# Last dense block of a fused attention and mixture-of-experts kernel: gate logits of its last five hidden tiles through a folded weight product, and their down matmuls in the first routing search

## The chip, the cores and the metric

One core of one Trainium2 chip. The metric is the device time of the whole kernel in microseconds (us); lower is better. TensorE (PE in the profile) does matrix products, VectorE (DVE) and ScalarE (ACT) elementwise work, GpSimd (POOL) indirect transfers and small tables, SyncE (SP) issues most DMAs.

## The reference, cut to what matters

```python
# x: 3072 tokens x 384, out of a linear-attention recurrence
h = np.maximum(x @ w_in, 0.0)             # dense block, w_in 384 x 2048
x2 = h * h @ w_out                        # w_out 2048 x 384
logits = x2 @ w_gate                      # 384 x 8
order = np.argsort(-logits.flatten())     # greedy assignment, every expert takes 384 tokens
for idx in order:
    tok, e = idx // E, idx % E
    if assigned[tok] >= 0 or counts[e] >= cap: continue
    assigned[tok] = e; counts[e] += 1
out[mask_e] = np.maximum(x2[mask_e] @ w1[e], 0.0) @ w2[e]     # w1 384 x 1024, w2 1024 x 384
```

The routing has to follow exactly computed logits, so every float32 operand of the big products is split into a high and a low part, and each product is three matmuls (high·high, high·low, low·high).

## The kernel before, in words

There are three stages. In the opening and the "blocks" the attention of chunk c runs beside the dense block of chunk c-1. Chunks have 128 positions of 4 sequences, so a dense block has 512 token columns; there are six (m = 0 to 5). A dense block is 16 hidden tiles of 128: `up(m, q, s)` is 9 matmuls into PSUM bank `U[s % 2]`, ScalarE takes the Relu (`hr`, line 725), VectorE squares it (line 953), ScalarE writes the high part `HH` (line 709) and VectorE the low part `HL` (line 965), both in rings of `HRING` = 4 tiles. `down(m, s)` is 9 matmuls into the three accumulators `ACC[0..2]`, `LAG` = 2 steps behind `up` (line 1448). Beside that, each step of the blocks c = 2 to 6 splits half a piece of an expert's weights into high and low (lines 709 and 973) and SyncE stores it to DRAM. `TERMS` lists the three parts of a product.

In the last call of `body` (c = 6, the dense block of chunk 5; `att` is false) steps 0 and 1 do `up(5, ., 0)` and `up(5, ., 1)` with the last two downs of the block before, and steps 2 to 15 do `up(s)` and `down(s - 2)`. The last two downs stand behind the body as a loop of its own (line 1476). At the steps 3, 5, 7 and 9 the rows of the block before are transposed (line 1417), and at step 3 its logits are computed (12 float32 matmuls with the 32 padded columns of `wg`, line 1379).

Then `ACC` goes to `x2T` by ScalarE and VectorE, `logits(0..2)` makes 12 float32 matmuls into `LAST_T`, VectorE copies them to `LT`, TensorE transposes them (line 1627), and VectorE takes them into `Lm` (line 1206). From there the first routing search runs (`r` = 0): for each of six levels of bits VectorE compares all keys with thresholds (line 1033), TensorE counts with 24 small bfloat16 matmuls (`count`, line 1506), VectorE finds which counts are full (line 1044), TensorE sums that (`digit_of`, line 1514), VectorE takes the digit and goes down a level. After the last level come `tie` (lines 1518, 1520), `owned` (1524), `slots` (1531) and the row indices `rowidx` (line 1141). Between these small steps TensorE is given matmuls without a use (`keep_warm`, line 1288; `warm_up`, line 1283) and the transposes of the last block's x2 rows, one of four for each level (`transpose_x2`, line 1483). ScalarE copies each and stores it with a DMA of its own queue to `x2_dram` (line 806, semaphores `st_last`).

GpSimd waits for `st_last` and for `rowidx`, then gathers expert 0's 384 rows in three indirect DMAs (line 676). TensorE transposes each (line 1541), they are split, and the expert's tiles begin (line 1572 for the first, 1595 and 1608 for the rest), with the later searches between them. SyncE waits for `st_last` (line 576), then for `widx` (which expert it is, line 1071), and loads that expert's pieces 0 and 1 of both parts; it then waits for all three gathers before pieces 3, 4 and 2. Expert 0's pieces go to the first 6144 columns of `WH` and `WL`, where the dense up weights were.

Of the kernel before, what the change touches and what calls it, by code (L numbers as in the profile page):

```python
# [53 lines left out]
MOST = NT - 6  # L54
TAB_STEPS = 18
# [9 lines left out]
def bass_attention_moe_routed_moe(nc, rk_in, tok_in, wT_in, urow_in, dw_in, w_gate, ew_in,  # L65
                                  tri_in, pcol_in, rows_in, masks_in, x2_dram, wh_dram, wl_dram, out):
# [19 lines left out]
    with ctx:  # L86
# [105 lines left out]
        x2last = [rk_flat[:, (CB + n) * DM:(CB + n + 1) * DM] for n in range(2)]  # L192
# [71 lines left out]
        acc_mm = sem("acc_mm")  # L264
        logit_mm = sem("logit_mm")

# [110 lines left out]

        def chunk_at(s, att, moe, post):
# [93 lines left out]
        LAST_T, LAST = U[0][:, 0:BATCH * EP], U[0][:, BATCH * EP:2 * BATCH * EP]  # L472
# [6 lines left out]
        def _(sp):  # L479
# [119 lines left out]
        def _(pool):  # L599
# [45 lines left out]
            pool.wait_ge(st_done, NT)  # L645
            pool.iota(iota, [[1, 128]], base=1, channel_multiplier=0,
# [60 lines left out]
        def _(act):  # L707
# [8 lines left out]
            def body(c, q, att, moe, post):  # L716
                m = c - 1
                for s in range(NF1):
                    if moe and post and s == LAG:
                        evacuate(m - 1)  # L720
                    if moe:
# [5 lines left out]
                        after(act, down_mm, g - HRING + 1)  # L727
                        copy(HH[:, s % HRING, :], hr[:, s % 2, :]).then_inc(hh_done, 1)
                    for n, kind, b in tasks_at(s, att, moe, post):
                        task(c, q, P[n % 3], kind, b)  # L730
# [66 lines left out]
            act.wait_ge(acc_mm, 1)  # L797
            copy(x2T[:, 0, :], ACC[0][:, :]).then_inc(acc_act, 1)
            act.wait_ge(acc_mm, 3)
            copy(x2T[:, 2, :], ACC[2][:, :]).then_inc(acc_act, 1)  # L800
            for b in range(BATCH):
                act.wait_ge(x2_mm, EARLY + b + 1)
                after(act, st_last[b % 2], 16 * (b // 2))
                copy(x2last[b % 2], x2_bank(b)).then_inc(row_done, 1)
                act.wait_ge(row_done, EARLY + b + 1)
                act.dma_start(x2_dram[b * SEQ + (NC - 1) * CHUNK:b * SEQ + NC * CHUNK, :],
                              x2last[b % 2]).then_inc(st_last[b % 2], 16)
# [45 lines left out]
        def _(dve):  # L853
# [91 lines left out]
            def body(c, q, att, moe, post):  # L945
                m = c - 1
                for s in range(NF1):
                    if moe and post and s == LAG:
                        evacuate(m - 1)
                    g = NF1 * m + s  # L950
# [5 lines left out]
                    for n, kind, b in tasks_at(s, att, moe, post):  # L956
                        task(c, q, P[n % 3], kind, b)
# [5 lines left out]
                    if moe:  # L963
                        dve.wait_ge(hh_done, g + 1)
                        tt(HL[:, s % HRING, :], hr[:, s % 2, :], HH[:, s % HRING, :].bitcast(f32),  # L965
                           ALU.subtract).then_inc(hl_done, 1)
                    if chunk_at(s, att, moe, post) is not None:
# [6 lines left out]
                    if moe and not att and s == 11:  # L974
                        dve.wait_ge(rt_go, 16 + NLEV)
                        nc.vector.tensor_copy(upperb, upper[:, :]).then_inc(tab, 1)
                        dve.wait_ge(lg_done, NC - 1)
# [221 lines left out]
            dve.wait_ge(x2_mm, EARLY)  # L1199
            dve.wait_ge(acc_mm, 2)  # L1200
            nc.vector.tensor_copy(x2T[:, 1, :], ACC[1][:, :]).then_inc(acc_dve, 1)
            dve.wait_ge(tab, TAB_STEPS + 1)
            dve.wait_ge(logit_mm, 1)
            nc.vector.tensor_copy(LT[:, :], LAST_T).then_inc(lt_done, 1)
# [71 lines left out]
        def _(pe):  # L1276
# [106 lines left out]
            def task(c, which, n, kind, b):  # L1383
                bank = P[n % 3]
                att, _, post = which
                if n >= 3:
                    evacuated(c, *tasks_of(*which)[n - 3][1:])
# [52 lines left out]
            def down(m, s):  # L1440
# [5 lines left out]
                for j in range(KT):  # L1446
                    for a, b in TERMS:
                        ins = mm(ACC[j][:, :], w_down((WH, WL)[a], s, j), (HH, HL)[b][:, s % HRING, :],  # L1448
                                 start=(s == 0 and a == b), stop=(s == NF1 - 1 and a == 1))
# [286 lines left out]
```

## Time and profile before

| | |
|---|---|
| Median of 3 runs | 810.31 us (808.18 to 811.10) |
| Profiled execution | 809.39 us, its span 807.6 us |
| TensorE busy | 791.7 us (98% of the span) |
| VectorE / ScalarE / GpSimd busy | 538.8 / 272.5 / 181.1 us |
| Mean granted TensorE clock | 0.999 |

Times inside the profile are counted from the start of the span. The 1.8 us between span and time lie around the span. "PEld" is the loading of stationary operands, which overlaps the matmuls; "SPq", "ACTq" and "POOLq" are DMAs being issued. The start times of matmuls that follow each other are the better measure of what one takes, since their ends are modelled and overlap. The last block of the dense stage runs to about 521 us, the first search from there to about 545 us, and expert 0 begins at about 553 us.

### The profile page before, as it was taken

To read this page: it belongs to the slowest core of one execution; us is meant where nothing else is said; L and a number is where in the kernel's file an instruction comes from. 1 tells how busy PE (TensorE), PEld (TensorE's weight loads), DVE (VectorE), ACT (ScalarE), POOL (GpSimd) and SP (SyncE) were. 2 spreads that over 40 slices of the span, in tenths; PEclk is the share of its full clock that TensorE was granted. 3 is DMA by queue.
4 is the path that set the end of the run, shared out by engine and by line. 5 is a ranking of instruction groups with operands and counts; after the bars stand their busy time and mean duration, and the time that the engine had idled before them with its cause. 6 is when DMAs were issued, how large, how long until landed. Compare 5 with 4: busy or idle time off the path is not lost.

```text
span 807.6 us, 16891 instructions
## 1 busy us (share of the span) xinstructions
PE 791.7 (98%) x6684; PEld 654.0 (81%) x6684; DVE 538.8 (67%) x1275; ACT 272.5 (34%) x513; POOL 181.1 (22%) x169
## 2 busy tenths in 40 slices
PE   8999999999999999999999999989999999999996
PEld 5677777777777778777777788748999999999996
DVE  7888757766767777777776445566867758667321
ACT  3543333334433343334333444301222122221321
POOL 5633232222122222222220300001122221231211
PEclk9999999999999999999999999999999999999999
DMA  8744226666666666666665556327466566664950
GB/s 281 229 134 134 83 95 212 207 208 222 209 204 224 197 209 212 211 212 212 215 212 168 187 187 205 132 96 262 150 225 238 198 229 203 229 250 145 350 208 30
DMA packets 62767, 157.75 MB, mean 195 GB/s; under 512 B 8288, under 2 KB 11616, under 8 KB 62688
## 3 DMA queue, kind: packets, MB, share of 16 engines
q1 hardware_dynamic: 56160, 142.51, 52.6%
q0 software_dynamic: 3072, 9.44, 3.6%
q10 hardware_dynamic: 3456, 4.72, 1.6%
q8 instruction: 53, 0.87, 0.5%
q14 instruction: 26, 0.21, 0.1%
HBM read 105.26 MB, written 51.38 MB: 194 GB/s over the span
## 4 chain that ended last, share of the span: by engine, by line
PE 87%; DVE 6%; DMA 2%; issue 2%; ACT 1%; POOL 0%; SPq 0%; POOLq 0%; DVEq 0%
PE ACC L1448 24%; PE U L1435 23%; PE U L1595 12%; PE ACC L1608 12%; PE P L1506 3%; PE P L1316 3%; PE P L1333 2%; PE P L1405 2%; PE P L1325 1%; DMA stage<-in_dw 1%; DVE WL L886 1%; PE P L1417 1%; DMA urow<-in_u 1%; DVE hr L953 1%; DVE HL L965 1%
## 5 line engine op out<-in xcount | busy, mean ns | idle before, releaser
L953 DVE TENSOR_TENSOR hr<-hr 128x512 f32<-128x512 f32 x96 | 67.2, 700 | 81.3 <-ACT hr L725 81.2
L1448 PE MATMUL ACC<-HH,WH 128*128 128x512 f32 x282 | 117.4, 416 | 0.0
L1435 PE MATMUL U<-XH,WH 128*128 128x512 f32 x288 | 114.1, 396 | 0.2 <-issue 0.2
L1435 PE MATMUL U<-XH,WL 128*128 128x512 f32 x288 | 113.9, 396 | 0.0
L1435 PE MATMUL U<-XL,WH 128*128 128x512 f32 x288 | 113.7, 395 | 0.0
L725 ACT ACTIVATE hr<-U 128x512 f32<-128x512 f32 x96 | 57.2, 596 | 161.0 <-PE U L1435 161.0
L1448 PE MATMUL ACC<-HL,WH 128*128 128x512 f32 x282 | 111.5, 395 | 0.0
L1448 PE MATMUL ACC<-HH,WL 128*128 128x512 f32 x282 | 111.3, 395 | 0.0
L709 ACT ACTIVATE HH<-hr 128x512 fp32r<-128x512 f32 x96 | 60.7, 632 | 94.1 <-DVE hr L953 92.6
L973 DVE TENSOR_TENSOR stage<-stage 128x512 fp32r<-128x512 f32 x80 | 70.0, 875 | 25.1 <-ACT stage L709 22.3
L965 DVE TENSOR_TENSOR HL<-hr,HH 128x512 fp32r<-128x512 f32 x96 | 71.7, 747 | 13.9 <-ACT HH L709 13.3
L833 ACT ACTIVATE HH<-U 128x384 fp32r<-128x384 f32 x64 | 31.5, 492 | 146.3 <-PE U L1595 143.4
L676 POOL DMA_INDIRECT rk<-x_rows,tok x24 | 26.5, 1104 | 200.2 <-DVE tok L1141 195.3
L1608 PE MATMUL ACC<-WL,HH 128*128 128x384 f32 x192 | 66.9, 349 | 0.0
L1595 PE MATMUL U<-XL,WH 128*128 128x384 f32 x189 | 66.4, 351 | 0.0
L1608 PE MATMUL ACC<-WH,HL 128*128 128x384 f32 x192 | 65.5, 341 | 0.0
L1608 PE MATMUL ACC<-WH,HH 128*128 128x384 f32 x192 | 65.4, 341 | 0.0
L1435 PEld LDWEIGHTS U<-XH,WH 128*128 128x128 f32 x288 | 54.1, 188 | 13.9 <-issue 0.6
L1595 PE MATMUL U<-XH,WL 128*128 128x384 f32 x189 | 65.2, 345 | 0.0
L1448 PEld LDWEIGHTS ACC<-HH,WH 128*128 128x128 f32 x282 | 52.9, 188 | 14.8 <-issue 1.4
L1435 PEld LDWEIGHTS U<-XH,WL 128*128 128x128 f32 x288 | 54.1, 188 | 13.2
L1435 PEld LDWEIGHTS U<-XL,WH 128*128 128x128 f32 x288 | 54.1, 188 | 12.9
(214 smaller groups left out, 1423.9 us busy)
## 6 DMA issues: line engine op xcount, KB each, us to landing
stage<-in_ew SPq DMA_DIRECT2D x80, 256.0 KB, 3.8
split_high<-stage SPq DMA_DIRECT2D x80, 256.0 KB, 2.1
split_low<-stage SPq DMA_DIRECT2D x80, 256.0 KB, 2.5
WH<-split_high SPq DMA_DIRECT2D x40, 512.0 KB, 5.8
WL<-split_low SPq DMA_DIRECT2D x40, 512.0 KB, 6.7
tok<-in_tok SPq DMA_DIRECT2D x24, 640.0 KB, 6.9
rk<-in_rk SPq DMA_DIRECT2D x22, 448.0 KB, 6.0
stage<-in_dw SPq DMA_DIRECT2D x8, 768.0 KB, 6.2
```

The lines of the kernel that those rows point to most:

```text
L676: pool.indirect_dma_start(out=xg[:, j, :], out_offset=None, in_=x2_dram[:, :], in_offset=bass.IndirectOffsetOnAxis(ap=rowidx[:, k, j:j + 1 ...
L709: return nc.scalar.activation(dst, src, ACT.Copy)
L725: nc.scalar.activation(hr[:, s % 2, :], U[s % 2][:, :], ACT.Relu).then_inc(relu_done, 1)
L833: nc.scalar.activation(HH[:, s % HRING, 0:CAP], U[s % 2][:, 0:CAP], ACT.Relu).then_inc(e_hh, 1)
L953: tt(hr[:, s % 2, :], hr[:, s % 2, :], hr[:, s % 2, :], ALU.mult).then_inc(sq_done, 1)
L965: tt(HL[:, s % HRING, :], hr[:, s % 2, :], HH[:, s % HRING, :].bitcast(f32), ALU.subtract).then_inc(hl_done, 1)
L973: tt(half_lo.bitcast(f32r), half_in[s % 2], half_hi, ALU.subtract).then_inc(half_lo_done, 1)
L1316: ins = mm(banks[par][:, p * 128:(p + 1) * 128], k_t[lo:lo + HDIM, p, :], r_t[lo:lo + HDIM, p, :], start=True, stop=True)
L1435: ins = mm(U[s % 2][:, :], w_up((WH, WL)[a], k, s), (XH, XL)[b][:, q, k, :], start=(n == 0), stop=(n == 3 * KT - 1))
L1448: ins = mm(ACC[j][:, :], w_down((WH, WL)[a], s, j), (HH, HL)[b][:, s % HRING, :], start=(s == 0 and a == b), stop=(s == NF1 - 1 and a == 1))
L1595: ins = mm(U[s % 2][:, 0:CAP], ew_up((WH, WL)[a], k % 2, t, s), (XHe, XLe)[b][:, k % 2, t, :], start=(t == 0 and a == b), stop=(t == KT - ...
L1608: ins = mm(ACC[j][:, 0:DM], (HH, HL)[a][:, s % HRING, j * 128:(j + 1) * 128], ew_down((WH, WL)[b], k % 2, s), start=(s == 0 and a == b), s ...
```

## The change

The logits are linear in the hidden tiles: `wg^T (Wdown^T H)` is `(Wdown wg)^T H`. The last block accumulates `ACC` only over its first 11 hidden tiles (`HELD`) and computes logits of that part from `x2T` as before. For the last 5 tiles (`KEPT`) the product of down weights and gate is made on chip (`fold_down`, from a second, transposed copy `dwt_in` of these weights, 983 KB, loaded by SyncE into the `tok` area in the block before), transposed (`fold_turn`), split, and multiplied with the hidden tiles (`folded`, 10 matmuls with a stationary operand of 64 columns). All add up in one bank `P[2]`; ScalarE copies its 96 partitions in two halves and four small matmuls with `by_group` (ones at equal remainders of 32) sum the groups and turn them at once. The 45 down matmuls of the five tiles stand in the first search in place of `keep_warm`, and the transposes and stores of the last rows, which need them, follow after `owned`.

So that the tiles stay there, the last block's hidden tiles from 4 on are written to free places (`hidden_tile`: 4 and 5 in `XH`/`XL`, 6 to 15 in the up-weight columns of `WH`/`WL` that are used up). SyncE waits for `acc_mm` = 3 before it loads expert 0's pieces over them. The X2 tasks of the last block use two PSUM banks in place of three, as `P[2]` is held. GpSimd's tables, which lie in the same `tok` area, wait for `fold_down`.

```diff
+KEPT = 5
+HELD = NF1 - KEPT
+LATE_MM = 3 * KT * KEPT
...
+        def hidden_tile(low, m, s):
+            if m == NC - 1 and s >= HRING + KT - 1:
+                at = (s - HRING - KT + 1) * BLK
+                return (WH, WL)[low][:, at:at + BLK]
+            if m == NC - 1 and s >= HRING:
+                return (XH, XL)[low][:, 0, s - HRING, :]
+            return (HH, HL)[low][:, s % HRING, :]
...
 SyncE
+                    if att and last and s == 9:
+                        sp.wait_ge(y_mm, BATCH * c + 2)
+                        sp.wait_ge(st_mm, BATCH * c + 2)
+                        sp.dma_start(area[:, 0:KT * KEPT * 128], dwt_in).then_inc(ld_down_t, 16)
...
+                if k == 0:
+                    sp.wait_ge(acc_mm, KT)
...
 GpSimd
+            pool.wait_ge(fold_mm, 1)
...
 ScalarE, last block
+                    if not att and s == NF1 - 1:
+                        act.wait_ge(down_mm, NF1 * m + HELD)
+                        copy(x2T[:, 0, :], ACC[0][:, :])
+                        copy(x2T[:, 2, :], ACC[2][:, :]).then_inc(acc_act, 1)
...
-            act.wait_ge(acc_mm, 1)
-            copy(x2T[:, 0, :], ACC[0][:, :]).then_inc(acc_act, 1)
-            act.wait_ge(acc_mm, 3)
-            copy(x2T[:, 2, :], ACC[2][:, :]).then_inc(acc_act, 1)
+            act.wait_ge(logit_mm, 1)
+            for n in range(2):
+                copy(LG_sum[:, n * BLK // 2:(n + 1) * BLK // 2],
+                     folded_sum[:, n * BLK // 2:(n + 1) * BLK // 2]).then_inc(sum_done, 1)
+            for k in range(KT):
+                act.wait_ge(acc_mm, k + 1)
+                copy(x2T[:, k, :], ACC[k][:, :]).then_inc(acc_act, 1)
...
 TensorE, last block
+                    if not att and s == 3:
+                        fold_down()
+                    if not att and s == 5:
+                        fold_turn()
+                    if not att and s >= LAG:
+                        if down_at(s) is not None:
+                            down(m, down_at(s))
...
+                return {3: 0, 4: 1, 6: 2, 7: 3, 8: 4, 9: 5, 10: 6, 11: 7, 12: 8, 13: 9, 14: 10}.get(s)
...
-            for s in (NF1 - 2, NF1 - 1):
...
+            for k in range(KT):
+                mm(P[2][EP * k:EP * (k + 1), :], wg[:, k, :], x2T[:, k, :], start=True, stop=False,
+                   skip_group_check=True)
+            pe.wait_ge(fold_l_done, 1)
+            pe.wait_ge(hl_done, NF1 * NC - 1)
+            for f in range(HELD, NF1 - 1):
+                for low in range(2):
+                    folded(f, low)
+            pe.wait_ge(hh_done, NF1 * NC)
+            folded(NF1 - 1, 0)
+            pe.wait_ge(hl_done, NF1 * NC)
+            folded(NF1 - 1, 1).then_inc(logit_mm, 1)
+            late_down(0, 2)
...
+            for b in range(BATCH):
+                pe.wait_ge(sum_done, 1 + b // 2)
+                ins = mm(LAST[:, b * EP:(b + 1) * EP], LG_sum[:, b * CHUNK:(b + 1) * CHUNK], by_group[0:KT * EP],
+                         start=True, stop=True)
+            ins.then_inc(logit_tr, 1)
...
             count(0, 0, range(LATE, NT), 0)
-            transpose_x2(0)
-            keep_warm(3, P[0])
+            late_down(2, 5)
+            at = 7
             for level in range(NLEV):
                 count(0, level, *(() if level else (range(LATE), 1, False)))
-                keep_warm(2, P[0])
+                late_down(at, 3 if level + 1 == NLEV else 2)
+                at += 3 if level + 1 == NLEV else 2
                 digit_of(0, level)
-                if level + 1 < BATCH:
-                    transpose_x2(level + 1)
-                keep_warm(2 if level + 1 < BATCH else 4, P[0])
-            keep_warm(1, P[0])
+                if level + 1 < NLEV:
+                    late_down(at, 5 if LEVEL_BITS[level + 1] > 5 else 4)
+                    at += 5 if LEVEL_BITS[level + 1] > 5 else 4
             tie(0)
-            keep_warm(3, P[0])
+            late_down(at, LATE_MM - at)
             owned(0)
-            keep_warm(12, P[0])
+            pe.wait_ge(acc_act, NC + KT)
+            for b in range(BATCH):
+                transpose_x2(b)
+            keep_warm(6, P[0])
             slots(0)
```

## Rows read from the trace of the kernel before

**Rows 1.** The page's chain that ended last: shares of the span by engine.

```profile
PE 87%; DVE 6%; DMA 2%; issue 2%; ACT 1%; POOL 0%; SPq 0%; POOLq 0%; DVEq 0%
```

**Rows 2.** The same chain in order of time: start, us, what ran.

```profile
512.81 2.10 PE U L1435 x9
...
517.01 4.22 PE ACC L1476 x18
...
612.30 4.65 DMA rk<-x_rows,tok
```

**Rows 3.** Waits in 455 to 515 us: us in total, times, longest.

```profile
PEld ACC L1448 <- issue: 0.6, 2, 0.4
```

**Rows 4.** Timeline (start, us, engine, line), last block, step 3.

```profile
461.93 0.49 PE L1417 MATMUL P<-tri,stage 128*128 128x128 f32 x3
...
462.36 0.86 PE L1379 MATMUL P<-stage,wg 128*32 128x128 f32 x24
```

**Rows 5.** Timeline from the last up tile to the logits in the table.

```profile
514.95 0.60 ACT L725 ACTIVATE hr<-U 128x512 f32<-128x512 f32 x1 [1.69 <-PE U L1435]
...
516.97 0.69 DVE L965 TENSOR_TENSOR HL<-hr,HH 128x512 fp32r<-128x512 f32 x1 [0.70 <-ACT HH L709]
...
519.85 0.60 ACT L709 ACTIVATE stage<-ACC 128x512 f32<-128x512 f32 x1 [2.39 <-PE ACC L1476]
...
522.81 0.33 PE L1627 MATMUL U<-tri,LT 128*128 128x128 f32 x1
...
523.17 0.19 DVE L1206 TENSOR_SCALAR Lm<-U 128x32 f32<-128x32 f32 x1 [0.42 <-PE U L1627]
```

**Rows 6.** Timeline of one level of the first search, TensorE.

```profile
529.43 0.77 PE L1506 MATMUL P<-tok 128*128 128x32 bf16 x24
...
530.04 0.59 PE L1288 MATMUL P<-onesb 128*128 128x512 bf16 x2
...
530.55 0.18 PE L1514 MATMUL P<-tok 128*128 128x8 bf16 x1
...
531.88 1.01 PE L1506 MATMUL P<-tok 128*128 128x64 bf16 x24 [0.33 <-DVE tok L1033]
```

**Rows 7.** Timeline: the ties' last matmuls and the slots' first.

```profile
539.67 0.38 PE L1520 MATMUL P<-tok 128*128 128x1 f32 x2 [0.24 <-DVE tok L1075]
...
544.32 0.78 PE L1531 MATMUL P<-tok 128*128 128x6 bf16 x24 [0.46 <-DVE tok L1136]
```

**Rows 8.** Timeline: the last x2 row's copy and store.

```profile
531.15 0.49 ACT L709 ACTIVATE rk<-ACC 128x384 f32<-128x384 f32 x1 [1.75 <-PE ACC L1483]
...
531.67 0.33 ACTq L806 DMA_DIRECT2D x_rows<-rk  x1
```

**Rows 9.** DMA issues in 500 to 600 us: x count, KB each, us to landing.

```profile
x_rows<-rk ACTq DMA_DIRECT2D x4, 192.0 KB, 1.9
```

**Rows 10.** Timeline: expert 0's choice, weights, gathers and first products.

```profile
539.11 0.15 DVE L1071 TENSOR_SCALAR tok<-tok 128x1 int32<-128x1 f32 x1
...
540.67 0.37 SPq L591 DMA_DIRECT2D WH<-split_high  x1
...
545.14 0.17 DVE L1141 TENSOR_REDUCE tok<-P 128x3 int32<-128x6 f32 x1 [0.40 <-PE P L1531]
...
546.30 1.25 POOL L676 DMA_INDIRECT rk<-x_rows,tok  x1 [95.04 <-DVE tok L1141]
...
549.18 1.00 POOL L676 DMA_INDIRECT rk<-x_rows,tok  x1 [0.30 <-issue]
...
552.56 0.52 PE L1541 MATMUL U<-tri,rk 128*128 128x128 f32 x3
...
561.22 0.34 PE L1608 MATMUL ACC<-WH,HH 128*128 128x384 f32 x1
```

**Rows 11.** Line 676 in 535 to 620 us: issue to landing, nine gathers.

```profile
DMA to landing us min/median/max: 3.1/3.1/4.7
```

**Rows 12.** Windows of GpSimd: us, busy, granted clock, DMA share, GB/s.

```profile
543.50:544.00 0.50, 0.00 (x0) 1.00 1.00 401
```

More of the change, by code:

```diff
@@ L726, in body @@
                         act.wait_ge(sq_done, g + 1)
-                        after(act, down_mm, g - HRING + 1)
-                        copy(HH[:, s % HRING, :], hr[:, s % 2, :]).then_inc(hh_done, 1)
+                        if att or s < HRING:
+                            after(act, down_mm, g - HRING + 1)
+                        copy(hidden_tile(0, m, s), hr[:, s % 2, :]).then_inc(hh_done, 1)
                     for n, kind, b in tasks_at(s, att, moe, post):
-                        task(c, q, P[n % 3], kind, b)
+                        task(c, q, task_bank(n, att), kind, b)
+                    if not att and s == 6:
+                        act.wait_ge(fold_mm, 2)
+                        copy(fold[:, :, 0, :], fold_turned.rearrange("p (n e) -> p n e", e=EP)).then_inc(fold_h_done, 1)
                     if chunk_at(s, att, moe, post) is not None:
@@ L949, in body @@
                         evacuate(m - 1)
+                    if not att and s == NF1 - 1:
+                        dve.wait_ge(x2_mm, EARLY)
+                        dve.wait_ge(down_mm, NF1 * m + HELD)
+                        nc.vector.tensor_copy(x2T[:, 1, :], ACC[1][:, :]).then_inc(acc_dve, 1)
                     g = NF1 * m + s
@@ L1197, in _ @@
             blocks(dve, body)
[L1199 to L1204, printed above, removed]
+            dve.wait_ge(tab, TAB_STEPS + 2)
             dve.wait_ge(logit_tr, 1)
@@ L1383, in task @@
             def task(c, which, n, kind, b):
-                bank = P[n % 3]
                 att, _, post = which
-                if n >= 3:
-                    evacuated(c, *tasks_of(*which)[n - 3][1:])
+                bank, banks = task_bank(n, att), 3 if att else 2
+                if n >= banks:
+                    evacuated(c, *tasks_of(*which)[n - banks][1:])
                 elif n == 0:
@@ new lines, in fold_turn, with folded @@
+            def fold_turn():
+                pe.wait_ge(fold_copied, 1)
+                nc.tensor.transpose(fold_turned[:, 0:128], fold_t[:, 0:128], ident[:, :])
+                nc.tensor.transpose(fold_turned[:, 128:KEPT * EP], fold_t[0:EP, 128:FCOLS],
+                                    ident[0:EP, 0:EP]).then_inc(fold_mm, 1)
+            def folded(f, low):
+                return mm(P[2][0:2 * EP, :], fold[:, f - HELD, :, :].rearrange("p a e -> p (a e)"),
+                          hidden_tile(low, NC - 1, f), start=False, stop=(f == NF1 - 1 and low == 1),
+                          skip_group_check=True)
@@ new lines, in late_down @@
+            def late_down(first, count):
+                for n in range(first, first + count):
+                    m = n - 3 * KT * (KEPT - HRING)
+                    term = n % 3
+                    if m < 0:
+                        f, j = HELD + n // (3 * KT), n // 3 % KT
+                    else:
+                        f, j = NF1 - HRING + m // 3 % HRING, m // (3 * HRING)
+                    a, b = TERMS[term]
+                    ins = mm(ACC[j][:, :], w_down((WH, WL)[a], f, j), hidden_tile(b, NC - 1, f),
+                             start=False, stop=(f == NF1 - 1 and a == 1), skip_group_check=True)
+                    if f == NF1 - 1 and a == 1:
+                        ins.then_inc(acc_mm, 1)
@@ L1623, in _ @@
                     SEQUENCE += [(e_down_mm, s - LAG, part, i) for part in range(CB) for i in range(3)]
-            keep_warm(2, P[0])
-            pe.wait_ge(lt_done, NC)
-            nc.tensor.transpose(LAST, LT[:, :], ident[:, :]).then_inc(logit_tr, 1)
+            pe.wait_ge(acc_act, NC)
+            pe.wait_ge(acc_dve, NC)
+            for k in range(KT):
+                mm(P[2][EP * k:EP * (k + 1), :], wg[:, k, :], x2T[:, k, :], start=True, stop=False,
+                   skip_group_check=True)
```

79 lines of the change are left out of this document (50 added, 29 removed).

## The prediction, as it was made before the changed kernel ran

> **What bounds the kernel now.** I read the page's chain first: 87% of the span is TensorE [rows 1]. So only what shortens TensorE's stream, or what it waits for, moves the time. The chain in order of time then gives the price of a tile: nine matmuls take 2.10 us, 0.233 each, and the last block ends with up 15, ended at 514.91, the down behind it, and the eighteen matmuls of line 1476 in 4.22 us [rows 2]. TensorE waits 0.6 us in all of that block [rows 3], so each down tile taken out of it is a full 2.10 us. From 521 on the picture turns: TensorE is kept busy with matmuls without a use, and the clock of the stage is a chain of small steps between VectorE and TensorE. The timeline shows what it starts with: the logits enter the table at 523.17, 8.26 us after the last up tile [rows 5]. Then come the levels of the search [rows 6], the ties and slots [rows 7], the row indices, the gathers of expert 0 and its first products [rows 10]. Those three parts are what the change touches.
>
> **The last block: -6.3 us.** In the body the last block had 14 downs, now it has 11: steps 2, 5 and 15 have none. That is 27 × 0.233 = 6.3 us before the last up tile ends. The two downs behind the body go as well, but they are counted in the third part, by the distance from the last up tile to the table. Cover that could be missing: a step without a down is 2.1 us of TensorE, and the chain Relu, square, high, low, half piece of the other engines is longer. In rows 5 Relu begins at 514.95 and the low part ends at 517.66, 2.7 us. But such steps stand alone between steps of 4.2 us, `up` needs only the Relu of two steps before, and the downs now come three or four steps late. I take nothing, with 0.5 us as upper end.
>
> **The fold: +1.6 us.** `fold_down` is 15 matmuls of 128 columns with 32 columns of weights. The same form ran 12 times (24 records) in 0.86 us [rows 4], so 15 take 1.1. The fifth tile of each round shares a column group with the first and might not overlap: up to 1.7. `fold_turn` is two transposes; three took 0.49 [rows 4], so 0.3. About 0.2 goes for entering and leaving. Its copies on VectorE and ScalarE (four of 0.3 us or less) lie a step ahead of their use, and the low parts are not needed for ten steps. The load of 983 KB is issued by SyncE in the block before. There it waits for products of unit 1 that are some steps old; behind it in SyncE's queue are the store and load of a half piece, which would be late by 983 KB at 401 GB/s [rows 12], 2.5 us, in a step of over 5 us. I take nothing, 0.5 at most. GpSimd's tables wait for `fold_down` but are used eight steps later: nothing. The X2 tasks have one bank fewer, and two steps between uses: nothing. Bounds of this part 1.3 and 2.9.
>
> **From the last up tile to the table: -3.5 us.** Before: 8.26 us. After, counted from the same end of up 15: the low part of tile 15 is there at 2.75 us [rows 5]. Meanwhile TensorE makes the logits of `x2T` (three float32 matmuls of 512 columns in three column groups). If they run side by side as in rows 4, each is four times a round of 128 columns (0.86 / 3 = 0.29), hence about 1.0 together; one after the other up to 2.6. `x2T` was copied during up 15, which covers ScalarE's two copies of 0.60 [rows 5]. Eight folded matmuls then end at 2.9, the ninth at 3.1, the last at 3.3, its result at 3.5. ScalarE copies 2 × 256 columns: 0.60 for 512 and 0.49 for 384 [rows 5, 8] give 0.38 each, to 4.3. Two small matmuls like the transpose of 0.33 [rows 5] bring the table to 4.75 us: 3.5 less than before. The ends: 3.7 if the low part alone decides, 1.9 if the three logit matmuls go one after another.
>
> **In the search: +0.4 us.** 45 late downs are 10.5 us of TensorE, put where useless matmuls and transposes were. A level has two slots. From count to digit two 512-column matmuls stood from 530.04 on, and the digit came at 530.55: 0.51 us [rows 6]. Two late downs take 0.47, and their float32 weights load longer than bfloat16. At the last level there are three, 0.70, so 0.2 over. From the digit at 530.55 to the next count at 531.88 are 1.33 us [rows 6]; five late downs take 1.17. So it fits, but by hundredths: I take 0.4 for all the levels, bounds 0 and 1.2.
>
> **The rows' stores move behind the search: +2.6 us.** This is what takes gain back. In the labels of before (so that only the new delay shows): the ties' last product begins at 539.67 [rows 7], ends at 540.05; three late downs end by 540.9; ScalarE's copy of the last `x2T` part (0.60) ends at 541.5; transposes by 542.05. This is ahead of the slots at 544.32 [rows 7], so TensorE loses nothing itself. But ScalarE must copy and issue four rows one after another: 0.49 for the copy, 0.33 for the issue, 0.15 between [rows 8], 0.97 each. The last store is issued at 545.5 and lands 1.9 later [rows 9], at 547.4. Before, the stores had all landed long before the row indices were ready at 545.31, and GpSimd's first gather began 0.99 us behind these [rows 10]. Now it begins at 548.4 in place of 546.30, 2.1 late. The third gather was issued at 549.18 and lands 3.1 later [rows 10, 11], at 552.3; its rows were turned at 552.56, so 0.3 was free. Alone, then, the delay is 1.85.
>
> They are no longer alone. SyncE waits for the same stores (line 576), which cost nothing while they were early: expert 0 was chosen at 539.26 and its first load issued at 540.67 [rows 10]. Now the load follows the landing by the same 1.4, at 548.8. Four loads of 512 KB at 401 GB/s [rows 12] move until about 555, over all three gathers. A gather beside weight loads took up to 4.7 in this kernel, 4.65 on the chain itself [rows 2, 11]: delay 3.4. The wait for `acc_mm` in the same queue is over by 540.9 and costs nothing. I take 2.6, between 1.85 and 3.4.
>
> The Trainium skill, "DMA: Bandwidth & Descriptors", Queues, rings and completion order, states that each DMA engine takes turns between queues packet by packet. By that the gathers get half the rate rather than stand behind all the weights, the delay would be an estimated 2.3 us; the 4.65 us row fits turns better than a full queue in front.
>
> **The sum.** -6.3 + 1.6 - 3.5 + 0.4 + 2.6 = -5.2 us. Against the profiled execution's 809.39 that is 804.2. The median of the runs is 0.9 above it; I put the forecast in the middle, 804.6. All small ends in one direction give -6.9 (802.5), all in the other about 0 (809.3 to 810).
>
> **Rivals.**
> Larger gain: gathers as fast as alone, search not stretched: -6.3 + 1.5 - 3.5 + 0 + 1.85 = -6.5, 802.9. For it: rows 6 leave room. Against it: the weights' new start.
> Smaller gain: the three logit matmuls go one after another (+1.6), or the search is stretched by 1.2, or gathers take 4.7: two of these give about -2.5, 807.3. For it: hundredths in rows 6, 4.65 in rows 2. Against: 12 products in 0.86 show that column groups overlap.
> No gain from the block: the last block runs at the pace of VectorE and ScalarE, so that the 6.3 is lost and the change doesn't do what it says: 804.6 + 6.3 = 810.9. Against it: 0.6 us of waits [rows 3] and Relu waiting 1.69 us for TensorE [rows 5].
> Slower: starved gathers and then TensorE's clock. If the weights' four loads went ahead of all gathers, these would land at 555 + 3 × 0.5 = 556.5 or later, TensorE would have little between 550 and 556, and its clock, granted at 1.00 (2.4 GHz) there [rows 12], could fall to 1.2 GHz. Before, 8.7 us lay between the third rows' transposes at 552.56 and the first down product at 561.22 [rows 10]; at half clock these cost up to 8.7 more. With a delay of 4.2 in place of 2.6 the change still gains 3.6; it decides from 3.6 us lost, thus 7.2 us at half clock, and the whole stretch gives +5.1, 814.9. Against it: warm-ups and a count stand between the gathers, and no row of this trace shows the lower clock.
>
> **How the numbers follow.** Forecast 804.6 (from 803.3 to 806): 0.45. Larger gain 0.15. Smaller gain 0.27. No gain from the block 0.06. Slower 0.07. The range 802.0 to 809.0 reaches from below the larger gain over the smaller one, and leaves out the last two and some tails. A difference under about 0.5% (4 us) can hardly be told from none by a measurement of this kernel. Faster by more takes most of the forecast's case and the larger gain: 0.58. Within 0.5%: some of the forecast's, the smaller gain, and most of no gain: 0.35. Slower by more: 0.07.
>
> **What would show each step.** Right: the last up tile ends about 4.7 us earlier (510.2); the table entry about 4.7 us behind it (515); levels as far apart as before; the first gather begins 8.7 us behind the ties' last product in place of 6.6, and is issued beside weight loads; TensorE waits for line 676 before line 1541. Wrong: a distance over 5.5 us from last up tile to table; levels stretched by over 0.1 us each; gathers landing in 3.1 us; a granted clock under 1 at about 545; or a wait of ScalarE for half pieces in the block before.

## The result and the profile after

| | before | after |
|---|---|---|
| Median | 809.56 us (12 runs, 808.18 to 811.10) | 811.09 us (12 runs, 810.53 to 813.00) |
| Ratio to before | 1 | 1.0022 [1.0012, 1.0032] |
| Profiled execution, its span | 809.39, 807.6 us | 811.04, 809.1 us |
| Mean granted TensorE clock | 0.999 | 0.991 |

The change costs 1.5 us (0.2%, with the interval clear of 1) where 5.2 us less were forecast. The page's chain of after, beside [rows 1], has more TensorE and more DMA on it:

```profile
PE 89%; DVE 5%; DMA 3%; issue 1%; ACT 1%; POOL 0%; SPq 0%; POOLq 0%; DVEq 0%
```

The same chain in order of time (start, us, what ran) shows where:

```profile
508.68 2.06 PE ACC L1507 x9
510.74 2.10 PE U L1494 x9
513.84 2.45 PE P L1530 x10
...
539.90 2.56 PE P L1347 x6
545.82 6.50 DMA rk<-x_rows,tok
```

The last up tile ends at 512.84, where before it ended at 514.91 [rows 2], and the eighteen down matmuls behind it are gone. New on the chain are six matmuls without a use (line 1347, the helper `keep_warm`) at 539.90, and a gather of expert 0 that takes 6.50 us; the one on the chain of before took 4.65 [rows 2]. The timeline of after from the last up tile to the ties (start, us, engine, line; in brackets the idle time before and what ended it), which answers to [rows 5 to 7]:

```profile
512.78 1.06 PE L1717 MATMUL P<-stage,wg 128*32 128x512 f32 x6
...
514.90 0.69 DVE L1019 TENSOR_TENSOR WL<-hr,WH 128x512 fp32r<-128x512 f32 x1 [0.70 <-ACT WH L749]
...
516.85 1.05 PE L1733 MATMUL U<-KW,AT 96*128 96x32 f32 x8
...
518.01 0.19 DVE L1265 TENSOR_SCALAR Lm<-U 128x32 f32<-128x32 f32 x1 [1.81 <-PE U L1733]
...
534.50 0.18 PE L1607 MATMUL P<-tok 128*128 128x1 bf16 x1 [1.29 <-DVE tok L1134]
...
534.91 0.38 PE L1609 MATMUL P<-tok 128*128 128x1 f32 x2 [0.24 <-DVE tok L1139]
```

and on to expert 0's first products, which answers to [rows 8 and 10]:

```profile
537.78 2.12 PE L1580 MATMUL ACC<-tri,stage 128*128 128x128 f32 x9
...
539.70 2.77 PE L1347 MATMUL P<-onesb 128*128 128x512 bf16 x6
...
541.23 0.33 ACTq L856 DMA_DIRECT2D x_rows<-AT  x1
...
542.26 0.79 PE L1620 MATMUL P<-tok 128*128 128x6 bf16 x24
...
544.26 1.26 POOL L716 DMA_INDIRECT rk<-x_rows,tok  x1 [72.09 <-DVE tok L1205]
...
544.65 0.37 SPq L630 DMA_DIRECT2D WH<-split_high  x1
...
550.33 0.52 PE L1630 MATMUL P<-tri,rk 128*128 128x128 f32 x3 [1.68 <-DMA rk<-x_rows,tok]
...
554.15 0.90 PE L1630 MATMUL U<-tri,rk 128*128 128x128 f32 x3
```

The logits are in the table 5.2 us earlier than before (518.01, [rows 5]: 523.17). But the third block of gathered rows is turned at 554.15, later than the 552.56 of [rows 10]. Two things are to be seen between. The first is the clock. Windows of after (us, busy time and count of TensorE, its weight loads, VectorE, ScalarE, GpSimd, then granted clock, DMA share, GB/s):

```profile
532.00:534.00 2.00, 1.21 (x19) 0.79 (x15) 0.91 (x7) 0.00 (x0) 0.00 (x0) 1.00 0.00 0
534.00:536.00 2.00, 1.26 (x6) 0.81 (x6) 1.84 (x13) 0.00 (x0) 0.00 (x0) 0.90 0.00 0
536.00:538.00 2.00, 1.42 (x7) 1.02 (x7) 1.40 (x8) 0.60 (x1) 0.00 (x0) 0.50 0.00 0
...
540.00:542.00 2.00, 2.00 (x6) 0.73 (x5) 0.00 (x0) 0.79 (x2) 0.00 (x0) 0.50 0.54 197
...
548.00:550.00 2.00, 0.66 (x11) 0.48 (x10) 1.38 (x4) 0.00 (x0) 0.32 (x1) 1.00 1.02 385
550.00:552.00 2.00, 1.08 (x13) 0.92 (x13) 0.56 (x1) 0.49 (x1) 0.00 (x0) 1.00 1.01 399
...
554.00:556.00 2.00, 2.00 (x20) 1.92 (x17) 0.52 (x2) 0.49 (x1) 0.00 (x0) 0.50 0.32 86
```

TensorE is at 0.50 (1.2 GHz, half of the upper level of 2.4) from 536 to 542 and again in 554 to 556 (0.67 over 552 to 554). The six matmuls of 512 columns then take 2.77 us, 0.46 each. The second is the DMA view of 545 to 556: the queues of the weights (q1) and of the gathers (q0) with packets, MB and share, and below, for line 716, the time from issue to landing:

```profile
q1 hardware_dynamic: 618, 2.27, 58.9%
q0 software_dynamic: 192, 0.59, 13.9%
```
```profile
DMA to landing us min/median/max: 5.9/6.5/6.8
```

[Rows 11] had a minimum and a median of 3.1 and a maximum of 4.7.

All that follows is counted from the entry of the logits into the table, since the opening, which no edit touches, differs between these traces: the table comes at 522.37 or 523.17 to 523.18 in kernels with before's last block, and at 516.40 to 516.58 or 517.89 to 518.10 in those with after's. "Third rows" is the start of the transposes of the third gathered block, "end" the end of the span.

| us after the table | ties' last product | slots | last x2 store issued | first gather | third rows | end |
|---|---|---|---|---|---|---|
| before | 16.50 | 21.15 | 8.50 | 23.13 | 29.39 | 284.43 |
| after | 16.90 | 24.25 | 23.22 | 26.25 | 36.14 | 291.09 |
| e1_warm | 16.90 | 21.55 | 22.54 | 26.67 | 36.74 | 291.90 |
| e7_before_cold | 16.47 | 22.19 | 8.49 | 24.15 | 31.51 | 286.52 |
| e4_before_late | 16.50 | 21.15 | 8.50 | 23.14 | 34.23 | 289.23 |
| e2_early | 16.88 | 23.92 | 23.27 | 31.64 | 38.62 | 293.17 |
| e3_both | 16.90 | 21.55 | 22.55 | 30.20 | 37.18 | 291.72 |
| e8_fill | 16.89 | 21.53 | 22.53 | 26.87 | 36.61 | 292.06 |
| e5_p0 | 16.88 | 21.53 | 22.54 | 27.40 | 34.35 | 289.10 |
| e6_p0_fill | 16.91 | 21.56 | 22.57 | 27.33 | 33.31 | 288.11 |
| e9_rows_first | 16.91 | 21.55 | 20.91 | 26.74 | 33.07 | 288.80 |

The first two lines give the balance. The last block is counted from the end of its first up tile, at 449.23 before and 450.05 after. From there to the table after is 5.98 us shorter (73.94 to 67.96). From the table to the end it is 6.66 longer: 0.40 up to the ties, 2.72 from there to the first gather, 3.63 from that to the third rows, and -0.09 behind them. Ahead of that point 0.82 is lost. -5.98 + 6.66 + 0.82 = 1.5, the difference of the spans.

### The profile page after: what moved, and what is told of

It is laid out like the page before. It is cut to its first block, busy times and chain, and to the rows that moved or that the text cites. A ratio compares the mean times of both kernels' runs of the same rounds, so it can differ in the third digit from the quotient of the medians.

```text
span 809.1 us, 16864 instructions
## 1 busy us (share of the span) xinstructions
PE 792.0 (98%) x6670; PEld 656.8 (81%) x6670; DVE 538.5 (67%) x1278; ACT 275.2 (34%) x519; POOL 177.4 (22%) x169
## 4 chain that ended last, share of the span: by engine, by line
PE 89%; DVE 5%; DMA 3%; issue 1%; ACT 1%; POOL 0%; SPq 0%; POOLq 0%; DVEq 0%
PE ACC L1507 23%; PE U L1494 23%; PE U L1684 13%; PE ACC L1697 12%; PE P L1595 3%; PE P L1375 3%; PE P L1392 2%; PE P L1464 2%; PE ACC L1544 1%; PE P L1384 1%; DMA stage<-in_dw 1%; DVE WL L936 1%; DVE hr L1007 1%; DMA urow<-in_u 1%; PE P L1476 1%
## 5 line engine op out<-in xcount | busy, mean ns | idle before, releaser
L1507 PE MATMUL ACC<-HH,WH 128*128 128x512 f32 x252 | 105.3, 418 | 0.0
L1507 PE MATMUL ACC<-HL,WH 128*128 128x512 f32 x252 | 99.7, 396 | 0.0
L1507 PE MATMUL ACC<-HH,WL 128*128 128x512 f32 x252 | 99.5, 395 | 0.0
L749 ACT ACTIVATE HH<-hr 128x512 fp32r<-128x512 f32 x84 | 53.1, 632 | 85.9 <-DVE hr L1007 85.9
L1019 DVE TENSOR_TENSOR HL<-hr,HH 128x512 fp32r<-128x512 f32 x84 | 63.3, 753 | 5.5 <-ACT HH L749 4.9
L749 ACT ACTIVATE stage<-stage 128x512 fp32r<-128x512 f32 x80 | 50.0, 625 | 42.2 <-DMA split_high<-stage 31.5
```

The source lines that it names most:

```text
L749: return nc.scalar.activation(dst, src, ACT.Copy)
L1019: tt(hidden_tile(1, m, s), hr[:, s % 2, :], hidden_tile(0, m, s).bitcast(f32), ALU.subtract).then_inc(hl_done, 1)
L1507: ins = mm(ACC[j][:, :], w_down((WH, WL)[a], s, j), hidden_tile(b, m, s), start=(s == 0 and a == b), stop=(s == (NF1 if m < NC - 1 else HE ...
```

## The experiments

The theory after this result: two prices were taken too small or not seen. (A) TensorE has too little to do around the ties, its clock falls, and the slots and the rows' stores come late. (B) Expert 0's gathers run beside its weight loads and are starved by them. The rivals: that only one of them counts, or that the half clock around the gathers, not the gathers, sets their pace.

Each ratio is to runs of the kernel before that were measured along with the run. Their median was 810.97 us for e1 to e4, 811.17 for e5 to e8 and 812.46 for e9, so the ratios can be compared and the medians can't. All differences are 0.6% or less.

### The clock around the ties

The change had taken out five 512-column matmuls ahead of the ties. `e1_warm` gives them back to after:

```diff
+            keep_warm(5, P[0])
             tie(0)
```

> The changed kernel with five useless 512-column matmuls put back between the last digit and the ties of the first search, as the kernel before had them. Theory W (the clock fell at about 535.9 us because TensorE had next to nothing to do between 533.0 and 534.5): the granted clock stays at 1.00 from 534 to 544, the 12 transposes take about 1.4 us in place of 3.1, the six useless matmuls 1.3 in place of 2.8, and the slots begin at about 540.2 in place of 542.26. But then the chain of ScalarE's four copies and stores is next: last store issued at about 540.7, landed at 542.7, first gather at about 543.6 in place of 544.26. So 0.7 to 1.1 us faster than the changed kernel, about 810.1. Rival N (the clock falls for a reason that lies elsewhere, such as the wait after the owned step): clock at half again from 536 on, time as the changed kernel, 811.1.

Measured: 811.57 us, 1.0018 [1.0005, 1.0031] of before. Windows and timeline of e1_warm, same columns as above:

```profile
534.00:536.00 2.00, 1.49 (x11) 0.99 (x10) 1.48 (x8) 0.75 (x2) 0.00 (x0) 1.00 0.00 0
536.00:538.00 2.00, 2.00 (x14) 1.11 (x12) 1.86 (x6) 1.20 (x3) 0.00 (x0) 1.00 0.27 98
```
```profile
538.05 0.77 PE L1620 MATMUL P<-tok 128*128 128x6 bf16 x24
```

The clock stays at 1.00 until past the slots, and these come at 21.55 instead of 24.25, close to before (21.15). Yet the first gather comes no earlier (26.67), for what is late next is the landing of the x2 stores. The last is issued at 22.54, only 0.7 earlier than in after, and it also takes longer to land. The chain of e1_warm, and below it the DMA view of 540.6 to 543 with the stores' queue (packets, MB, share):

```profile
539.04 3.06 DMA x_rows<-AT
```
```profile
q10 hardware_dynamic: 9, 0.01, 2.5%
```

In after the four stores landed in 1.8 to 1.9 us each. Here the last took 3.06 (3.27 in e8), and from 540.6 on only nine packets of the stores moved, with nothing beside them. Why is not shown. So the clock was a real delay of the slots, 2.7 us. But with it gone the stores hold the gather: by when they are issued it could have come about 0.7 us earlier, and the slow landing of the last one took that away.

`e7_before_cold` does (A) alone to the kernel before:

```diff
-                keep_warm(2 if level + 1 < BATCH else 4, P[0])
-            keep_warm(1, P[0])
+                if level + 1 < NLEV:
+                    keep_warm(2 if level + 1 < BATCH else 4, P[0])
```

> The kernel before with the five useless matmuls between the last digit and the ties of the first search taken out, nothing else. Theory W (these five are what held the clock there): the clock falls to half within a few us behind the ties; the twelve useless matmuls behind the owned step then take 5 us in place of 2.75 and the slots start about 2 us late, 23.2 us behind the table's entry in place of 21.15; 2 us slower than the kernel before, 0.25%. Rival: the clock stays at 1.00 because the three and twelve useless matmuls behind the ties are enough, and the time is the same; then it took in the changed kernel the absence of those too.

Measured: 812.43 us, 1.0012 [1.0001, 1.0024]. Windows of e7_before_cold:

```profile
538.00:540.00 2.00, 0.52 (x4) 0.44 (x5) 1.82 (x15) 0.00 (x0) 0.00 (x0) 1.00 0.00 0
540.00:542.00 2.00, 1.65 (x8) 0.52 (x6) 1.48 (x8) 0.00 (x0) 0.00 (x0) 0.79 0.21 51
542.00:544.00 2.00, 2.00 (x6) 0.63 (x5) 1.83 (x6) 0.00 (x0) 0.00 (x0) 0.50 0.88 289
544.00:546.00 2.00, 2.00 (x31) 1.23 (x30) 0.71 (x2) 0.00 (x0) 0.00 (x0) 0.86 0.96 250
```

Five matmuls less are enough to lose the clock: TensorE is busy for 0.52 of 2.00 us and the next windows are at 0.79 and 0.50. The slots come 1.04 late and the end 2.1 in the profile, about 1 us by the ratio. The slots were forecast at 23.2 and came at 22.19: VectorE is busy for 1.83 of 2.00 us in 542 to 544, so its steps probably still fill most of the distance.

### The gathers beside the weight loads

`e4_before_late` does (B) alone to the kernel before: expert 0's loads wait until the row indices are there, so that they start beside the first gather.

```diff
+                if k == 0:
+                    sp.wait_ge(idx_done, 1)
```

> The kernel before with one wait added: SyncE waits for expert 0's row indices before it loads pieces 0 and 1, so that they are issued 0.4 us behind the first gather, as in the changed kernel; nothing else differs. Theory G: gathers up to 6.8 us, third transposes about 3.6 us late, and 3.6 to 4.1 us slower than the kernel before, about 813.4. Rival S (the stores just before are what slows the gathers): gathers in 3.1 us, the only cost is piece 0 landing at about 549.5, before its use at 553.4, hence no change, 809.6.

Measured: 814.83 us, 1.0054 [1.0037, 1.0071]. Timeline, the gather on the chain and one window of e4_before_late:

```profile
545.51 1.43 POOL L678 DMA_INDIRECT rk<-x_rows,tok  x1 [95.05 <-issue]
...
545.96 0.37 SPq L593 DMA_DIRECT2D WH<-split_high  x1
...
556.60 0.88 PE L1543 MATMUL U<-tri,rk 128*128 128x128 f32 x3
```
```profile
547.25 7.32 DMA rk<-x_rows,tok
```
```profile
552.00:554.00 2.00, 1.69 (x13) 1.36 (x12) 0.70 (x2) 0.49 (x1) 0.00 (x0) 0.50 1.01 387
```

The first gather is as early as in before (23.14), the third rows are 4.84 us later, and the end is 4.80 later. This is the price of the collision with nothing else changed, the clock's fall that it brings included. Rival S is out: the last store was issued 16 us before this 7.32 us gather (530.87, 547.25).

`e2_early` takes the weights off the gathers in after: the waits for `st_last` and `acc_mm` move down, so that pieces 0 and 1 load as soon as the expert is known.

```diff
-            for i in range(2):
-                sp.wait_ge(st_last[i], 16 * BATCH // 2)
...
-                if k == 0:
-                    sp.wait_ge(acc_mm, KT)
                 for n in (0, 1, 3, 4, 2):
+                    if k == 0 and n == 3:
+                        sp.wait_ge(acc_mm, KT)
+                        for i in range(2):
+                            sp.wait_ge(st_last[i], 16 * BATCH // 2)
```

> The changed kernel, but SyncE loads pieces 0 and 1 of expert 0 as soon as its number is known, and waits for the last stores and for the late downs only before piece 3 (pieces 0 and 1 lie where tiles 6 to 9 were, which no late down reads). Theory G (the gathers took up to 6.8 us because four weight loads of 512 KB ran beside them): loads issued at about 536, gathers land in 3.1 us again, the third transposes come 6.3 us behind the first gather as in the kernel before, about 550.5 in place of 554.15, the second fall of the clock at 553 goes too, and the time is 3.6 to 4.1 us below the changed kernel's, about 807.2, faster than the kernel before by 2.4. Rival S (gathers are slow because they follow the stores of the same rows too closely, the weights don't matter): gathers 6 us again, time 811 or a little more.

Measured: 811.93 us, 1.0023 [1.0011, 1.0035]. This was a miss of mine. The DMA issues of e2_early in 534 to 556 (KB each, median us to landing) say why:

```profile
x_rows<-rk ACTq DMA_DIRECT2D x2, 192.0 KB, 7.0
x_rows<-AT ACTq DMA_DIRECT2D x2, 192.0 KB, 7.7
```

The loads now run over the rows' stores, and these land after 7.0 and 7.7 us in place of 1.9 [rows 9]. The first gather slips to 31.64. From it to the third rows are 6.98 us, against 9.89 in after: the gathers are free of the loads (the first lands in 3.31 us on the chain), and all of it is paid ahead of them. That is 0.7 more than the 6.3 forecast, and the clock is at 0.50 in 550 to 554.

`e3_both` is e1 and e2 together.

> Both edits together. If theories W and G hold and their costs add, 0.7 to 1.1 plus 3.6 to 4.1 us: about 806.3, 3.3 below the kernel before. If the low clock also hid something in the early loads, less; if the first gather is bound by the stores' landing in both, the first edit adds at most 0.7 to the second.

Measured: 811.57 us, 1.0007 [0.9996, 1.0018], a miss of the 806.3 as well. First gather at 30.20, third rows at 37.18: the clock restored, stores and weights still collide, and the gathers are as late as that makes them.

`e8_fill` asks whether (B) is the gathers or the clock that falls while TensorE waits for them. It is e1 with sixteen useless matmuls in the wait:

```diff
+            keep_warm(16, P[0])
             transpose_rows(0, 0)
```

> The changed kernel with the five useless matmuls before the ties and sixteen (3.4 us at full clock) in the wait for the first gather, weight loads left where the change has them, beside the gathers. It takes the clock out of the price of that collision. If gathers alone set the pace, the third transposes stay 36.7 us behind the table as without the fill, the first tiles behind them run at full clock and the end is 0.5 to 1 us earlier. If the half clock was most of that price, over 2 us earlier.

Measured: 811.29 us, 1.0008 [0.9993, 1.0023]. e1_warm and then e8_fill in the window in which e1 waits for the gather:

```profile
546.00:548.00 2.00, 0.00 (x0) 0.00 (x0) 0.00 (x0) 0.00 (x0) 1.16 (x2) 0.50 0.88 336
```
```profile
546.00:548.00 2.00, 1.83 (x9) 0.63 (x7) 0.00 (x0) 0.00 (x0) 1.18 (x2) 1.00 1.01 348
```

The clock holds at 1.00 until 552, and still the third rows come at 36.61 (e1: 36.74). The pace is that of the gathers; the half clock beside them hid in their wait. The end was forecast 0.5 to 1 us earlier and is not (292.06, e1: 291.90): from 552 on the clock fell in e8 too (0.76, 0.50, 0.88), so what a full clock would be worth behind the gathers is not separated by this kernel.

### Between the two collisions

`e5_p0` loads only piece 0 of expert 0 early and holds the rest back until the gathers have landed. It starts from e1, with the waits as in e2, but at `n == 1`, and

```diff
-                    if n == (3 if k < NE - 1 else 0):
+                    if n == (1 if k == 0 else 3 if k < NE - 1 else 0):
```

> The changed kernel with the five useless matmuls before the ties, and with SyncE's order changed: piece 0 of expert 0 (two loads, 1 MB) as soon as its number is known, before the stores of the last rows; the waits for late downs and stores and gathers, and then piece 1 and the rest, behind. So neither the last stores nor the gathers have weight loads beside them, but for the first store or two. Theory G (bulk loads beside small dependent transfers are what costs): stores land as in the first run with the five matmuls (first gather 26.7 us behind the logits' entry into the table) or 0.5 us later, gathers land in 3.1 us, the third transposes 6.3 us behind the first gather, that is 33.2 behind the table in place of 36.1 in the changed kernel and 29.4 before. The whole is 2.5 us faster than the changed kernel and 1.5 faster than the kernel before (ratio 0.998). Rival D (a delay of the stores' own, at about 200 GB/s, and of piece 1 needed by the third up tile, take its place): third transposes no earlier than 35, time as the changed kernel.

Measured: 808.92 us, 0.9967 [0.9953, 0.9980]. The third rows come 6.95 us behind the first gather, where e1 had 10.07, and at 34.35 behind the table where 33.2 was forecast. The end is 2.8 earlier than e1's. The stores, beside 1 MB now, land in 3.7 and 3.8 us.

`e6_p0_fill` adds to it what e8 added to e1, with 8 matmuls.

> The same with eight useless 512-column matmuls more before the first gathered rows are turned, 1.7 us at full clock, in the time in which TensorE waits for the gather. Theory W: the granted clock stays at 1.00 where it fell to half at about 545 in the runs so far; the three transposes and the count between them lose nothing, so 0.5 to 1 us less than without the fill, ratio to the kernel before 0.997. If the gathers alone set the pace, no difference to the kernel without the fill.

Measured: 807.84 us, 0.9969 [0.9956, 0.9982]. The clock is at 1.00 in every window to 558 and the third rows come another 1.0 us earlier; the two ratios can't be told apart. Chain of e6_p0_fill:

```profile
540.46 3.70 DMA x_rows<-AT
```

The chain now goes through the landing of the last x2 row. `e9_rows_first` therefore gets the stores out earlier: the last late downs stand ahead of the ties, three of the transposes of `x2T` ahead of `owned`, and the fourth behind it. Against e6:

```diff
-            keep_warm(5, P[0])
-            tie(0)
             late_down(at, LATE_MM - at)
-            owned(0)
+            keep_warm(2, P[0])
+            tie(0)
...
-            for b in range(BATCH):
+            for b in range(BATCH - 1):
                 transpose_x2(b)
-            keep_warm(6, P[0])
+            owned(0)
+            transpose_x2(BATCH - 1)
+            keep_warm(8, P[0])
```

> The run with piece 0 early and the gather wait filled, and the last three late downs moved ahead of the ties (with two useless matmuls in place of five), so that the rows' first three transposes stand ahead of the owned step. Theory G says that what is left of the loss is the chain of the four stores, since slots are at 21.6 us behind the table and the first gather at 27.3. Last store issued 20.9 us behind the table in place of 22.6, first gather at 25.7 in place of 27.3, third transposes at 31.7 in place of 33.3, table to end 286.5 in place of 288.1, clock 1.00 throughout: ratio to the kernel before 0.995, beating both kernels. Rival: the stores then meet piece 0's loads in full and land no earlier (the four move at 200 GB/s beside 400 GB/s of loads), first gather at 27 again and the ratio 0.997; or the owned step is held up by the transposes and the search is longer by what the stores gain.

Measured: 808.57 us, 0.9952 [0.9935, 0.9969], the best ratio of all. The last store is issued at 20.91, 1.7 earlier than in e6, but the first gather comes only 0.6 earlier, at 26.74, and the end not at all (288.80). DMA issues of e9_rows_first in 534 to 562, and its chain behind the gathers:

```profile
x_rows<-AT ACTq DMA_DIRECT2D x2, 192.0 KB, 5.0
```
```profile
553.05 7.56 DMA WL<-split_low
```

The stores have moved into piece 0's loads: 5.0 in place of 3.8 in e6. And the chain now goes through the low part of expert 0's piece 3, issued at 553.05 behind piece 1, which itself was held back for the gathers. The distance from the third rows to the end is 255.73 us, 0.93 more than in e6. This is what the rival D of e5_p0 warned of, weights that come too late, though for another piece. That e9 is better than e6 is not shown; the intervals of e5, e6 and e9 overlap. All three are faster than before, by 0.3 to 0.5%, and their intervals lie below that of after.

## Why the prediction was wrong

**The last block, -6.3 +1.6: a tile counted twice.** The mechanism held. TensorE sets the pace, also through the steps without a down. In the waits of after in 455 to 512 us (us in total, times, longest) Relu waits for TensorE and not the other way round:

```profile
ACT hr L769 <- PE U L1494: 13.9, 11, 1.7
```

But before, down 13 stands behind up 15. Ahead of the end of the last up tile only 13 downs stood, and 11 stand there after: 2 × 2.1 = 4.2, not 6.3. The prediction's own [rows 2] had it: up 15 ends at 514.91, the eighteen matmuls begin at 517.01, and the 2.10 between are down 13. These 2.10 are in the 8.26 us of the next part, and were taken off there once more. The fold was sized right. Its stretch in after's timeline:

```profile
460.82 0.86 PE L1438 MATMUL P<-stage,wg 128*32 128x128 f32 x24
461.50 1.47 PE L1516 MATMUL P<-tok,wg 128*32 128x128 f32 x30
462.90 0.50 PE L1507 MATMUL ACC<-HH,WH 128*128 128x512 f32 x1
```

`fold_down` takes 1.40 us from its start to the next down. Between the end of `up` and the start of the down (nine starts at a pace of 2.10 us) stand 1.22 us at step 3 before and 2.50 after; with the slower matmul behind them that is 1.29 more. At step 5, with `fold_turn`, it is 0.47 more: 1.76 together for a forecast of 1.6. -4.2 + 1.76 = -2.4; measured -2.9 (65.68 to 62.79 us from the end of the first up tile). Of the 0.5 left, 0.26 is a wait around the down of step 2, which is gone with it, and 0.20 are the last five downs, which take 2.06 us each in place of 2.10.

**From the last up tile to the table, -3.5: measured -3.09.** 5.17 us in place of 4.75. The three logit matmuls run side by side, 1.06 us for a forecast of 1.0, and the low part of the last tile begins at 2.06 and ends at 2.75 behind the up tile, as said. What was under-sized is the end: the four small matmuls of line 1733, of which two were counted, at the price of one transpose of 0.33, take 1.05 together (8 passes in the row).

Here the prediction had weighed a rule. In the rows the passage from 128 to 32 columns of weights costs little: the matmul of 512.78 begins 0.33 us behind the last one of 128 columns, at a pace of 0.23. The tail is 0.4 us over, nearly all of it in line 1733. The Trainium skill, "TensorEngine Tiling (Array Packing)", Key Properties, says that a change of tiling mode drains TensorE, from which the prediction had an estimated 1 us for the whole. The 0.10 us beyond the pace at 512.78 may be such a drain; no run here separates it.

**The search, +0.4: measured +0.40.** Two late downs a slot fit as costed, and 0.29 of the 0.40 fall into the last level, which has three. But the step was read for time alone. In the same stretch five useless matmuls ahead of the ties went, and the step did not ask what these held up: the clock (e7).

**The stores behind the search, +2.6: measured +6.35.** Three terms.

First, the stretch to the first gather was forecast at +2.1 and came to +2.72. The forecast said that TensorE loses nothing there; it lost the clock, and in after the gather waits for the row indices behind the late slots (543.26; the last store had landed at about 543.1). e7 and e1 show the cause. The chain of stores that the forecast went by was sized well up to the last issue (5.64 us behind the ties' last product in e1, 5.8 forecast). Its landing was put at 1.9 and took 3.06 in e1, so that with the clock held the stretch is +3.14, no shorter. With a landing of 1.9 it would be about +2.0, close to the forecast.

Second, and this is the step that failed most, the gathers beside the weight loads: forecast +0.5, bounded by one row of 4.65 us; they landed in 5.9 to 6.8, and +3.63 was paid. e4 measures the collision alone at +4.84. The bound was also misread. The prediction took the 4.65 us for a gather beside weight loads, but the DMA view of before in 610.5 to 617 has the gathers (q0) and nothing beside them:

```profile
q0 software_dynamic: 192, 0.59, 32.5%
q1 hardware_dynamic: 2, 0.00, 0.2%
```

So no row that the prediction used shows a gather that meets four starting loads, and its bound of 3.4 was no bound. Third, the weights' later start itself was seen correctly: loads issued 0.4 us behind the first gather. Behind the third rows nothing more is lost (-0.09).

By the Trainium skill, "DMA: Bandwidth & Descriptors", Queues, rings and completion order, each DMA engine takes turns between queues packet by packet, from which the prediction had an estimated delay of 2.3 us for the whole step. The case comes out worse: the DMA view has 192 packets of gathers and 618 of weights, and by turns the gathers would wait for 192 of the 618. That is 0.7 MB, an estimated 1.8 us at 399 GB/s, and e4 measured 4.84. The 4.65 us row, which the prediction held for a sign of turns, had no loads beside it and says nothing about turns.

**The rivals.** The mechanism of the slower one came true: starved gathers, TensorE with little to do, clock at 1.2 GHz. Its row against, "warm-ups and a count stand between the gathers", did not help: in after TensorE is busy for 0.66 and 1.08 of 2.00 us in the two windows of 548 to 552. Its price was over-sized, as the half clock lay mostly in the wait (e8) and nothing more was lost behind the third rows. And its list of places left out the first fall, at the ties.

**In sum.** -5.2 forecast, +1.5 measured, also outside the range (802.0 to 809.0). Of the 6.7 between, 2.2 are block and tail (the tile counted twice, less 0.3 in the block, and 0.4 in line 1733), 3.75 the stores and gathers, and 0.8 the opening.

**Open.** The opening's 0.82 lies in code that the change does not touch, and other traces of the same code differ by up to 1.5 us there; no kernel tested it. How the DMA engines divide themselves between gathers and loads was measured, not explained, and why the last store of e1 and e8 landed late is not known. Not settled is also which of e5, e6 and e9 is fastest.

## What to carry to other kernels

When work goes off the critical path, count its tiles by where each stands in the order, and let each stretch of the trace be in one term only. When useless matmuls are replaced by useful ones, check the granted clock behind each gap that is left, above all where TensorE waits for VectorE. A transfer that used to be early has neighbours: put down what each queue holds at its new place, and expect a short gather or store beside bulk loads to take two to four times its own time. Before a row serves as a bound for such a collision, check in the DMA view what ran beside it.

## What the runs showed of the hardware

- Gathers of 128 rows landed in 3.1 us at the median of nine in before, and in 4.7 at most, that one with no loads beside it. Beside four loads of 512 KB that start with them they took 5.9 to 6.8 us (after) and 7.32 (e4).
- Stores of 192 KB with no loads beside them land in 1.8 to 1.9 us, the last of four once in 3.06 (e1) and once in 3.27 (e8). Beside 1 MB of loads they take 3.5 to 5.6 (e5, e6, e9), beside 2 MB 6.6 to 8.1 (e2, e3).
- Ahead of the first fall of the clock to 0.50 TensorE had been busy for 1.21 and 1.26 of two windows of 2.00 us, with a gap of 1.29 across their border (after), and for 0.52 of 2.00 in e7. At 0.50 a useless 512-column matmul takes 0.46 us, at 1.00 0.24 (six in 1.46, e1). The Trainium skill, "TensorE: Matmul & The Clock Gate", What's actually happening, names 1.2 and 2.4 GHz as the two levels; the traces agree, with 0.50 and 1.00 for whole windows.
- Three float32 products of 512 columns in three groups of 32 columns take 1.06 us together; in sequence they would take 2.6 by the prediction's working.
